# Moving two tiles of the second network by 416 bytes: turned rows up, rounded activations down

## The reference

```
h = x @ w_in                  # 384 -> 2048
g = maximum(0.01 * h, h)
out = g @ w_out               # 2048 -> 384
```

## Time and profile before

| | us |
|---|---|
| median of 3 runs | 817.96 |
| lowest and highest | 816.58, 819.44 |
| the profiled execution | 815.64 |
| its span, first to last instruction | 813.8 |
| TensorE busy | 799.8 |
| VectorE busy | 450.8 |
| ScalarE busy | 344.6 |

### The profile page before, as it was taken

How to read it: one execution, slowest core, us unless ns; L and a number is a source line. 1 busy time by engine, 2 the same in 40 slices (tenths; PEclk the granted TensorE clock), 3 DMA queues, 4 the chain that set the end, 5 groups by cost and what they waited for, 6 DMA issues and landing times.

```text
span 813.8 us, 17577 instructions
## 1 busy us (share of the span) xinstructions
PE 799.8 (98%) x5259; PEld 719.6 (88%) x5260; DVE 450.8 (55%) x705; ACT 344.6 (42%) x643; POOL 208.0 (26%) x278
## 2 busy tenths in 40 slices
PE   7999998999999999999999999999999999999998
PEld 7888877888989989989989898998989898998987
DVE  7899987686567476566565333423433432433332
ACT  3555564566446256444353342333333333324223
POOL 6676722223333343341232021003004001001000
PEclk9999999999999999999999999999999999999999
DMA  9987763767888887897741110201201001000001
GB/s 234 275 249 235 226 224 103 253 208 262 304 281 268 301 271 225 286 298 244 194 57 19 22 39 1 40 1 39 39 0 39 0 0 39 1 1 19 21 1 39
DMA packets 64130, 108.98 MB, mean 134 GB/s; under 512 B 24199, under 2 KB 45747, under 8 KB 64080
## 3 DMA queue, kind: packets, MB, share of 16 engines
q1 hardware_dynamic: 54896, 93.47, 37.4%
q0 software_dynamic: 5888, 14.85, 5.7%
q10 hardware_dynamic: 3296, 0.06, 0.2%
HBM read 78.89 MB, written 30.85 MB: 135 GB/s over the span
## 4 chain that ended last, share of the span: by engine, by line
PE 90%; DVE 3%; DMA 2%; issue 2%; POOL 1%; DVEq 0%; ACT 0%; SPq 0%; ACTq 0%; POOLq 0%
PE bank L1772 25%; PE bank L1721 24%; PE bank L1694 14%; PE bank L1674 14%; PE bank L1516 3%; PE bank L1556 3%; PE bank L1533 2%; PE bank L1564 1%; PE bank L1522 1%; PE bank L1650 1%; DMA xg<-x_rows,isrc 1%; PE bank L1576 1%; DMA qkas<-qka 1%; POOL kt L675 1%; DVE decay L1073 1%
## 5 line engine op out<-in xcount | busy, mean ns | idle before, releaser
L1721 PE MATMUL bank<-yT,wts 128*128 128x512 f32 x864 | 209.8, 395 | 0.3 <-DVE g L1302 0.3
L1772 PE MATMUL bank<-wts,gs 128*128 128x384 f32 x1152 | 207.2, 334 | 0.0
L1772 PEld LDWEIGHTS bank<-wts,gs 128*128 128x128 f32 x1152 | 201.0, 188 | 4.3
L1721 PEld LDWEIGHTS bank<-yT,wts 128*128 128x128 f32 x864 | 161.4, 188 | 35.5 <-DVE g L1302 0.7
L1302 DVE TENSOR_TENSOR g<-bank,small 128x512 f32<-128x512 f32 x96 | 65.9, 687 | 171.9 <-ACT small L929 155.9
L1674 PE MATMUL bank<-wts,gxT 128*128 (+1 forms) x549 | 133.7, 396 | 0.2 <-issue 0.2
L929 ACT ACTIVATE small<-bank 128x512 f32<-128x512 f32 x96 | 57.3, 597 | 164.3 <-PE bank L1721 145.5
L1674 PEld LDWEIGHTS bank<-wts,gxT 128*128 128x128 f32 x549 | 100.8, 188 | 21.3 <-issue 1.1
L1483 DVE TENSOR_TENSOR gs<-g,gs 128x512 fp32r<-128x512 f32 x96 | 66.5, 693 | 66.7 <-ACT gs L1034 64.2
L1034 ACT ACTIVATE gs<-g 128x512 fp32r<-128x512 f32 x96 | 60.7, 632 | 83.6 <-DVE g L1302 76.5
L774 POOL DMA_INDIRECT out<-os,tokens x20 | 19.7, 986 | 283.7 <-ACT os L1023 279.2
(11 more groups left out here) (179 smaller groups left out, 779.8 us busy)
## 6 DMA issues: line engine op xcount, KB each, us to landing
raw<-weights SPq DMA_DIRECT2D x60, 512.0 KB
hidden_rows<-hs SPq DMA_DIRECT2D x29, 512.0 KB
hds<-hidden_rows SPq DMA_DIRECT2D x29, 512.0 KB
qkas<-qka SPq DMA_DIRECT2D x20, 675.5 KB, 5.4
vs<-v SPq DMA_DIRECT2D x24, 192.0 KB, 4.3
x_rows<-xs SPq DMA_DIRECT2D x24, 192.0 KB, 3.9
yl<-y_rows SPq DMA_DIRECT2D x20, 192.0 KB
qkas<-qka SPq DMA_DIRECT2D x4, 227.5 KB, 6.1
```

Of the source, the lines that this page charges most:

```text
L1721: m = pe.matmul(gps[f % 2][:, :], wts[:, 0, w_part, n:n + P], yT[:, 1 - u, y_part, k], start=(k == 0 and (w_part, y_part) == (0, 0)), stop ...
L1772: m = pe.matmul(ops[tt], gs[:, f % 4, g_part, tt * P:(tt + 1) * P], wts[:, 1, w_part, f * D:(f + 1) * D], start=(f == 0 and (g_part, w_par ...
```

## The change

A helper `seat(by)` lays a filler tile so that the next tile begins `by` bytes after `wts`, modulo 512. It is called before `yT` (256) and before `os_` (352). The filler before `yT` comes to 416 bytes; the one before `os_` to 96, so `os_`, `hT_odd`, `tokens` and `row_gates` end up 512 bytes higher. `hds` and `hr` move with `yT`. `gs` is placed 416 bytes lower. Instructions, waits and transfers are the same in number and order.

```diff
--- before.py
+++ after.py
@@ -49,6 +49,7 @@
     GT = TG * P
     GROUPS = N // GT
     FT = F2 // P
+    LINE, TO_W_IN, FROM_W2 = 512, 256, 352
     HT = F // P
     HALF = F // 2
 
@@ -182,6 +183,13 @@
             def sb(name, shape, dt=F32):
                 return phase.enter_context(nc.sbuf_tensor(name, shape, dt))
 
+            def seat(by):
+
+                here = (nc.sbuf_base + 31) // 32 * 32
+                gap = (wts_at + by - here) % LINE
+                if gap:
+                    sb(f"gap{here}", [P, gap // 4])
+
             xg_at = (nc.sbuf_base + 31) // 32 * 32
             xg = sb("xg", [P, 2, D])
             gxT = sb("gxT", [P, 2, 2, D], F32R)
@@ -193,6 +201,7 @@
             idst = sb("idst", [P, 2], I32)
             yl = sb("yl", [P, 2, GT // SQ, PIECE])
             yf = sb("yf", [P, 2, GT])
+            seat(TO_W_IN)
             yT_at = (nc.sbuf_base + 31) // 32 * 32
             yT = sb("yT", [P, 2, 2, KD, GT], F32R)
 
@@ -200,6 +209,7 @@
             hds = nc.alloc_sbuf_tensor_at("hds", [P, 2, F], F32, offset=yT_at)
             hr = nc.alloc_sbuf_tensor_at("hr", [P, 2, HALF], F32, offset=yT_at + 2 * F * 4)
             assert 3 * F <= 2 * KD * GT
+            seat(FROM_W2)
             os_at = (nc.sbuf_base + 31) // 32 * 32
             os_ = sb("os", [P, 2, TG, D])
 
@@ -210,8 +220,8 @@
 
             small = nc.alloc_sbuf_tensor_at("small", [P, 2, GT], F32, offset=xg_at)
             g = nc.alloc_sbuf_tensor_at("g", [P, 2, GT], F32, offset=xg_at + 2 * GT * 4)
-            gs = nc.alloc_sbuf_tensor_at("gs", [P, 4, 2, GT], F32R, offset=hs_at)
-            assert hs_at == xg_at + 2 * D * 4 + 4 * D * 4 and 4 * GT * 4 <= hs_at - xg_at and 8 * GT == 4 * F
+            gs = nc.alloc_sbuf_tensor_at("gs", [P, 4, 2, GT], F32R, offset=hs_at - 416)
+            assert hs_at == xg_at + 2 * D * 4 + 4 * D * 4 and 4 * GT * 4 <= hs_at - 416 - xg_at and 8 * GT == 4 * F
         hps = [[bank[2 * j + r] for r in range(2)] for j in range(2)]
         htps = [bank[4], bank[5]]
         yeps = [bank[6][:, 0:D], bank[4][:, 0:D]]
```

## The result

| | before | changed | ratio |
|---|---|---|---|
| median, 7 runs each (us) | 816.89 | 812.68 | 0.9953 (95%: 0.9937 to 0.9969) |
| the profiled execution | 815.64 | 812.94 | |
| its span | 813.8 | 810.9 | |

The forecast was 812.3. Faster by 0.5% is what was measured: 4.2 us between the medians, 3.8 us by the ratio, with an interval of 2.5 to 5.1 us (0.31% and 0.63% of 816.89). The time was met more closely than the mechanism, as the trace shows, and more closely than the saving: with seven runs the kernel before stands at 816.89, 1.1 us under the 817.96 that the forecast started from, and the saving is some 1.4 us short of the 5.6. The two errors nearly cancel, which is luck.

The account below looks back on a forecast made before the run. TensorE, busy 98% of the span, was taken as the bound. 5.5 us from the loop and 0.12 from early runs, with 0 for the activations and the tiles moving along, took 817.96 to 812.3 us; range 809.8 to 816.5.

Parts of the forecast that it names:

- TensorE's spacing goes into the end one to one: In the loop from 430 us on, a changed matmul spacing enters the end time fully, with no wait between.
- Part 1: Inner matmuls (L1721), rows' distance 160 to 256: spacing 233.3 to 226.7 ns, runs 4.20 to 4.08 us, 5.6 us saved.
- register work: In L1674's hidden blocks, it was taken to explain 4.21 us for 18; L1721's loop has none, so the steady row counted.
- The term of 5.5 us: Steady stretch of the loop: 46 inner runs of 18, each 0.12 us shorter, give 5.5 us.
- a partial gain: Inner matmuls (L1721): spacing of 228 to 231 ns, time 813.5 to 816 us; chance 0.03.
- Part 2: Outward matmuls (L1772), activations' distance 256 to 352: no difference, 1152 x 0 = 0, bounds 0.5 us either way.
- steady part: Of hT_even (L1694) at distance 256: 17 matmuls in 2.95 us, 173.5 ns each, taken as its spacing.
- Part 3: Tiles that move along (hds, hr, os and others): cost 0, at most some hundredths where the stages meet.
- The sum: 5.5 us from the loop's steady stretch plus 0.12 from early runs, 5.6 us; median 817.96 to 812.3.
- Rival 1: No change, 818.0 us: L1721's dearer spacing comes from something other than the distance, or needs another distance; chance 0.11.
- Rival 2: Larger gain: the new place also removes the spacing's fixed part or some of it, down to 801 us; chance 0.02.
- Rival 3: Slower, 820.0 us: the cost at 352 moves from L1721 to L1772, 7.7 us come against 5.6 gone; chance 0.04.

Follow-up runs that it names:

- with 400: The changed kernel with the activations 48 bytes higher, 400 from w_out in place of 352; median 810.73 us, ratio to before 0.9937.
- three comparisons: The changed kernel measured against the kernel before three times; ratios 0.9953, 0.9961 and 0.996.
- the sweep: The kernel before plus a weights-only series, inner distance swept 0 to 480 by 32; 36 matmuls take 8.20 us at 256, 8.40 at 352.

## Why the prediction was right, and where not

- **TensorE's spacing goes into the end one to one.** Right within the noise. The changed kernel and those with the rows alone and with 400 have pairs of 8287, 8307 and 8260 ns and save 3.4 (mean of three comparisons), 2.1 and 5.1 us by their ratios; 46 pairs make 3.4, 2.4 and 4.6 us. With the activations alone it is 2.5 lost against 1.8. No wait appeared in the loop.
- **Part 1, the rows.** Right in mechanism, wrong in size. The steady rate at 256 is 226.7 ns, as the experts' rows said. The failed step is the reading of the rows of L1674: I took the second half of a block as the price and put its dear first half down to "register work". The loop has none, and the opening is there: 38 ns a run. The number was in the earlier trace rows: 18 matmuls in 4.21 us, which I held to be a bound and didn't believe. Its excess of 134 ns over 18 x 226.7 had two parts: 87 in the first matmul after a turn of rows (314 ns), and 47 in the same kind of decay that the changed loop shows. The trace of before even has one such block with no turn of rows ahead of it, though by the code its register work is the same:

```profile
387.19 4.29 PE L1674 MATMUL bank<-wts,gxT 128*128 x18
```

  To the next run at 391.32 it takes 4122 ns, against 4118 in the changed loop. So the first matmul is dear only behind a turn (what part register work has in it there, no run tells), and this whole run at 256 was the witness to take. The term of 5.5 us measures 46 x 0.082 = 3.8. As a mean spacing that is 4118 / 18 = 228.8 ns, which belongs to the case of a partial gain (228 to 231 ns) that was given 0.03.
- **Part 2, the activations.** Forecast 0, measured 46 x 8 ns = 0.4 us of loss beside the kernel before. But "no difference" was the wrong reading. Both old rows were right for their own neighbours only. Moving the rows to 256 by itself takes the outward run from 4160 to 4186 ns, and moving the activations to 352 then takes 18 of these 26 back, with 2 or 3 more on the inner run: 20 ns a pair (8307 to 8287, 0.9 us in all). Given the rows at 352, the same move costs 40. The term came out near nothing because of this loss and gain, and not because the two distances are alike. The rows held a warning: at one and the same distance of 256, L1772 took 4.16 us for 24 and hT_even 399.67 - 395.48 = 4.19, and the "steady part" left out the seven matmuls that made the difference (177 ns each).
- **Part 3.** Right: VectorE's 672 and 669 ns are 674 and 671 after, its subtraction into gs stays at 693, and ScalarE's rounding at 631 to 632.
- **The sum.** 5.6 us forecast. By the ratios the three comparisons give 3.8, 3.2 and 3.3, by the medians 4.2, 4.0 and 4.0, and the trace's loop 3.4 (3.8 less 0.4). That 812.3 came so near 812.68 is owed to the start at 817.96, as said above.
- **Rival 1** is refuted by the sweep: equal matmuls of one tile and one line run at 226.7 or 233.3 ns by the distance of their operands. The Trainium skill, "TensorE: Matmul & The Clock Gate", section "Step-by-step: what each phase is for", says that the next load doesn't take read bandwidth from the running matmul. These runs don't agree with what the prediction drew from that, that no distance could matter, and the measurement decides; whether what the two reads share is bandwidth, they don't show.
- **Rival 2**: nothing came under 226.7 ns as a lasting rate for 512 columns, in any of the sweeps' settings.
- **Rival 3**, the cost moving over to w_out, didn't happen, but it was nearer than the 0.04 said: at 352 the outward line does have a dear pattern (4.24 us), and only the inner run ahead of it keeps it out. hT_odd was no full witness, as it followed a run at 256.

## What to carry to other kernels

When TensorE is the bound and every matmul loads new weights, read the spacing from start to start before looking anywhere else, and compare equal shapes within the kernel; a steady rate lower by 6.7 ns for 512 columns was worth 3.8 us here, openings included, for an edit of addresses alone. Take the price of a run from whole runs, openings included, not from its steady part, and doubt an explanation (here register work) that lets you drop the dear half until a row shows it. Where two placements act on each other, sweep them as a pair in a series behind the kernel: each of two runs priced sixteen settings, and together they gave again the pairs of three kernels already measured and foresaw that of the fourth (8259 ns, measured 8260).

## What the runs showed of the hardware that was not expected

- The distance between stationary and moving operand acts with a period of 256 bytes (36 matmuls agree to 1 ns at all eight pairs of distances), and for runs of 512 columns of float32r and weights of 128 columns one point in eight (by 32) settles at 226.7 ns, the others at 228.9 to 234.3.
- At the same distance, what ran ahead changes a run: at 256 it decides between openings of 0 and 31 ns for 24 matmuls (4160 to 4191 in the sweep), and at 352 between lasting spacings of 173.3 and 176.6 ns.
- Half the weight columns, with half the output's partitions, don't mean half the loss: 0.26 to 0 us at one distance, 0.04 to 0.12 at another, for 36 matmuls.
